# Expert rows in tiles of 128 + 96, the 96 as 32-column matmuls four side by side, and h's bound from sums that the relu accumulates

## The chip, the cores and the metric
The kernel runs on one core of one Trainium2 chip. Its time is the device time of an execution in microseconds (us). Engines are named as the profile names them: PE (TensorE), ACT (ScalarE), DVE (VectorE), POOL (GpSimd), SP (SyncE). They run side by side and wait for each other by semaphores only.

## The reference
Attention over 4 x 12 heads of 448 tokens gives x with 1792 rows of 768. A feed-forward layer (2048 wide, squared relu) gives y. A gate assigns each of the 1792 tokens to one of 8 experts, in order of falling logits, each expert taking exactly 224 rows. The part that changes is the last one:

```
for e in range(E):                      # E = 8
    mask = assigned == e                # 224 rows
    h = np.maximum(x[mask] @ w1[e], 0.0)    # 224 x 768 by 768 x 1024
    out[mask] = h @ w2[e]                   # 224 x 1024 by 1024 x 768
```

## The kernel before
Every float32 product is made of three float16 ones: an operand is scaled by a power of two, rounded (its hi part, on ACT) and the rest kept (its lo part, on DVE), and hi*hi + hi*lo + lo*hi is summed in PSUM. A scale needs a bound of the operand over all partitions, which POOL forms by a reduction over partitions (L656 to L667).

The expert stage is a loop that every engine writes out by itself: `step(e)` for e = -2, -1 and 0, a hardware loop for 1 to 5, then 6 and 7. Each engine's queue is in order. A turn overlaps three experts:
- PE (`step` at the end): `expert_up(e+1)`, L1742, 4 groups of 36 matmuls of 224 columns, each group followed by a relu; `expert_down(e, 0)` and `(e, 1)`; `turn_rows(e+2)`, 12 transposes; `expert_down(e, 2)` and `(e, 3)`. A down job, L1756, is 24 matmuls of 384 columns. The 224 rows are two tiles of 112, so job j is row tile j // 2 and column half j % 2. From its third group on, up waits for the relu two groups back, since it has two banks. A down needs all lo parts of h and of w2.
- ACT: `eh_hi(e)` (L850, after expert e-1's downs), `w2_hi(e)` (L859) with the relus of expert e+1 (L891) between, `w2_abs(e+1)` (L884, sums of w2's absolute values), `rows_out(0)` (L908, PSUM to the output tile), `w1_hi(e+2)` 0 and 1 (L866), `rows_out(1)`, `w1_hi` 2, `rows_hi(e+2)` (L871), `w1_hi` 3, `rows_out` 2 and 3.
- DVE: the lo parts `eh_lo(e)` (L1405) and `w2_lo(e)` (L1359); the absolute maximum of w1 of expert e+2 (L1354) and its scale (L343 to L355); the maximum of all of h of expert e+1 (L1436), which is read once POOL has reduced it, and its scale; `w1_lo(e+2)` 0 to 2 (L1364), `rows_lo(e+2)` (L1369), `w1_lo` 3; w2's scale (L1374 and three more); the output's scale o_inv (L1399). For expert 0 the maximum of h is taken in four parts (L1420), one per relu.
- POOL: the gather of expert e+2's rows (L650), the reductions for w1, w2 and h (L658, L661, L667), and two scatters of 112 output rows each (L674), one per row tile. SP loads w1 and w2, 3 MB each, two turns ahead.

The last expert's h and w2 parts lie where w1's were, so `eh_hi(7)` and `w2_hi(7)` don't wait for expert 6's downs: ACT does `rows_out(0)`, `eh_hi(7)`, `w2_hi(7)` 0 and 1, `rows_out(1)`, `w2_hi(7)` 2 and 3:

```
rows_out(0)
if is_last(e + 1):
    eh_hi(e + 1)
    w2_hi(e + 1, 0, 1)
...
rows_out(1)
if is_last(e + 1):
    w2_hi(e + 1, 2, 3)
```

Two earlier places matter for the prediction: the gate's matmuls (L1577) have 32 columns of weights and write four quarters of the partitions in turn, and one kind of tile in the layer before (L1651) has pairs of 64 columns.

Of the kernel before, what the change touches and what calls it, by code (L numbers as in the profile page):

```python
# [53 lines left out]
QK_ROWS = (TP, 128)  # L54
BEHIND = 2
# [11 lines left out]
def build(nc, q_d, k_d, v_d, cap_d, win_d, wout_d, wgate_d, w1_d, w2_d, out_d, y_d):  # L67
    with ExitStack() as ctx:
# [70 lines left out]
        grid = lambda: take(CH * E).rearrange("p (c e) -> p c e", e=E)  # L139
        masked, best, pick, newly, place = grid(), grid(), grid(), grid(), grid()  # L140
# [13 lines left out]
        low_hot = take(CH * TP // 2, F16).rearrange("p (c q) -> p c q", c=CH)  # L154
        group_hot = take(CH * CH).rearrange("p (c g) -> p c g", c=CH)
# [17 lines left out]
        lows = take(TP)  # L173
        grid_i = take(TP, I32)
# [24 lines left out]
        w1_sums, w1_tops, w2_sums, w2_tops, eh_parts_max, eh_tops = (take(4) for _ in range(6))  # L199
# [46 lines left out]
        BANK_E1, BANK_E2, BANK_ET = 0, 2, 4  # L246
# [31 lines left out]
        s_E2, s_o, s_oi, s_idx, s_sct, s_free = sem("expert_down"), sem("out_rows"), sem("out_inv"), sem("out_index"), sem("out_written"), sem("out_rows_free")  # L278
# [291 lines left out]
        def _(pool):  # L570
# [32 lines left out]
            pool.iota(grid_i, [[1, TP]], base=0, channel_multiplier=0).then_inc(s_rt, 1)  # L603
# [38 lines left out]
            def gather_rows(e):  # L642
                hold(s_tT, 3 * e)
                pool.tensor_copy(row_idx[0:TP], ids[0:TP, bass.ds(2 * e, 2)]).then_inc(s_gidx, 1)
                hold(s_gidx, e + 1)
                if first(e):
                    for t in range(NTILE - 4, NTILE):
                        hold(s_yw[t % 4], y_written(t))
                for c in range(2):
                    pool.indirect_dma_start(out=yg[0:TP, c, :], out_offset=None, in_=y_d[:, :],  # L650
                                            in_offset=bass.IndirectOffsetOnAxis(ap=row_idx[0:TP, c:c + 1], axis=0)).then_inc(s_ygl[c], 16)

            def step(e):
# [8 lines left out]
                if expert_live(e + 1):  # L662
                    hold(s_em, 1 if first(e + 1) else e + 3)
                    if first(e + 1):
                        pool.partition_all_reduce(eh_tops, eh_parts_max, 128, RMAX).then_inc(s_ea, 1)
                    else:
                        pool.partition_all_reduce(eh_amax, eh_max, 128, RMAX).then_inc(s_ea, 1)  # L667
                if expert_live(e):
                    pool.tensor_copy(idx[0:TP], ids[0:TP, bass.ds(2 * e, 2)]).then_inc(s_idx, 1)
# [12 lines left out]
        def _(act):  # L682
# [155 lines left out]
            def step(e):  # L838
# [64 lines left out]
                def rows_out(j):  # L903
                    if expert_live(e):
# [3 lines left out]
                        act.activation(e_out[0:TP, j // 2, (j % 2) * (DM // 2):(j % 2 + 1) * (DM // 2)],  # L908
                                       psum[0:TP, BANK_E2 + j % 2, 0:DM // 2], ACT.Copy, scale=o_inv[0:TP]).then_inc(s_o, 1)
# [30 lines left out]
        def _(dve):  # L940
# [255 lines left out]

            total = [0]
# [147 lines left out]
            dve.tensor_copy(ids[0:TP], psum[0:TP, BANK_IDS, 0:CH]).then_inc(s_ids, 1)  # L1345
# [5 lines left out]
            def step(e):  # L1351
# [66 lines left out]
                def part_max(j):  # L1418
                    dve.wait_ge(s_ER, 2 + j + 1)
                    return dve.tensor_reduce(eh_parts_max[:, j:j + 1], eh[:, j * 2 * CAP:(j + 1) * 2 * CAP], AX.X, ALU.max)  # L1420

                if first(e + 1):
                    part_max(0)
                    w1_lo(e + 2, 0)
                    part_max(1)
                    rows_lo(e + 2)
                    w1_lo(e + 2, 1)
                    part_max(2)
                    w2_lo(e + 1, 0)
                    part_max(3).then_inc(s_em, 1)  # L1430
                    dve.wait_ge(s_ea, 1)
# [356 lines left out]
```

## Time and profile before

| | us |
|---|---|
| median of 3 runs (lowest, highest) | 1068.84 (1066.81, 1070.94) |
| the profiled execution | 1069.31 |
| its span | 1067.6 |
| attention, feed-forward and routing, up to about | 798 |
| from the first gather to up(0) | 801 to 810.7 |
| expert loop, turns 1 to 5, each | 30.6 |
| last down, start to end | 1043.87 to 1059.66 |

A row of a timeline is start, duration, engine, line and operation, what it writes and reads, how many instructions are merged, and in brackets the idle time in front of it and what ended it. Durations of single matmuls include the fill of the array; what a matmul costs in a stream is read from the starts.

### The profile page before, as it was taken

The numbers are of one execution on the slowest core, as the hardware profiler recorded it, in microseconds if no ns is written. First come the engines' busy times: TensorE is split into PE (matmuls) and PEld (weight loads), VectorE is DVE, ScalarE is ACT, GpSimd is POOL, SyncE is SP. The second block draws the span as 40 slices with busy tenths as digits, with TensorE's granted clock in tenths as the row PEclk, the third lists the DMA queues.
The fourth block names the chain that finished last, engine by engine and source line by source line (L and its number), as shares of the span: only waits on it lengthen the run. The fifth ranks groups of instructions, "written<-read, shape, count | busy, mean of one in ns | idle before, by whom it ended". The sixth has DMA issues, their size and how long they took to land.

```text
span 1067.6 us, 23565 instructions
## 1 busy us (share of the span) xinstructions
PE 1029.5 (96%) x8700; PEld 748.3 (70%) x8700; DVE 819.5 (77%) x1699; ACT 588.9 (55%) x942; POOL 197.2 (18%) x319
## 2 busy tenths in 40 slices
PE   6999999999999999999999999999987999999996
PEld 3444444444469999999976666666656889888895
DVE  5899998999967656665686667666678899999971
ACT  5888887898846233333461111313215688877791
POOL 3444443444320000000000000000001132212211
PEclk9999999999999999999999999999997999999999
DMA  3752211121034000000241040401048566677401
GB/s 93 206 148 54 66 54 52 53 60 53 18 110 137 2 1 2 2 1 2 90 150 31 16 149 16 149 16 31 16 148 278 179 234 231 249 270 286 158 14 52
DMA packets 66782, 103.44 MB, mean 97 GB/s; under 512 B 14480, under 2 KB 44432, under 8 KB 66704
## 3 DMA queue, kind: packets, MB, share of 16 engines
q1 hardware_dynamic: 64144, 91.34, 26.0%
q0 software_dynamic: 2560, 11.01, 3.4%
q8 instruction: 54, 0.88, 0.4%
q14 instruction: 24, 0.20, 0.1%
HBM read 91.32 MB, written 11.01 MB: 96 GB/s over the span
## 4 chain that ended last, share of the span: by engine, by line
PE 79%; DVE 11%; issue 5%; DMA 2%; ACT 1%; POOL 1%; DVEq 0%; SPq 0%; POOLq 0%; ACTq 0%
PE psum L1465 21%; PE psum L1648 17%; PE psum L1756 10%; PE psum L1742 8%; PE psum L1510 5%; PE psum L1495 4%; PE psum L1519 4%; DVE arena L1030 3%; PE psum L1651 3%; PE psum L1681 2%; DMA arena<-y_rows,arena 1%; PE psum L1539 1%; DVE arena L1022 1%; PE psum L1724 1%; PE psum L1577 1%
## 5 line engine op out<-in xcount | busy, mean ns | idle before, releaser
L1465 PE MATMUL psum<-arena 128*128 128x224 f16 x2304 | 224.2, 259 | 1.0 <-DVE arena L1002 1.0
L1465 PEld LDWEIGHTS psum<-arena 128*128 128x128 f16 x2304 | 219.8, 98 | 5.3 <-issue 2.4
L1648 PE MATMUL psum<-arena 128*128 128x384 f16 x1152 | 195.9, 326 | 0.0
L1648 PEld LDWEIGHTS psum<-arena 128*128 128x128 f16 x1152 | 107.7, 98 | 66.9 <-issue 0.8
L590 POOL TENSOR_SCALAR arena<-arena 128x448 f32<-128x448 f32 x168 | 105.4, 638 | 162.0 <-DVE arena L1012 161.9
L1756 PE MATMUL psum<-arena 128*112 128x384 f16 x768 | 127.1, 326 | 0.4 <-issue 0.4
L723 ACT ACTIVATE arena<-arena 128x448 f32<-128x448 f32 x168 | 125.6, 750 | 1.0 <-DVE arena L1032 1.0
L805 ACT ACTIVATE arena<-psum,arena 128x384 f32<-128x384 f32 x28 | 16.2, 580 | 186.5 <-PE psum L1648 144.4
L1742 PE MATMUL psum<-arena 128*128 128x224 f16 x1152 | 114.0, 262 | 3.8 <-DVE arena L1390 2.0
L1756 PEld LDWEIGHTS psum<-arena 128*112 128x112 f16 x768 | 99.3, 130 | 24.8 <-issue 0.7
L1742 PEld LDWEIGHTS psum<-arena 128*128 128x128 f16 x1152 | 111.5, 99 | 6.0 <-DVE arena L1390 2.4
L716 ACT ACTIVATE arena<-psum,arena 128x896 f32<-128x896 f32 x96 | 87.5, 912 | 45.8 <-PE psum L1495 27.9
L738 ACT ACTIVATE arena<-psum 128x448 f32<-128x448 f32 x64 | 34.7, 543 | 136.0 <-PE psum L1465 136.0
L1519 PEld LDWEIGHTS psum<-arena 128*128 128x128 f32 x576 | 61.9, 142 | 62.7 <-issue 37.5
L1495 PE MATMUL psum<-arena 64*128 64x448 f32 (+1 forms) x336 | 100.1, 603 | 4.9 <-ACT arena L716 2.2
L1030 DVE TENSOR_REDUCE arena<-arena 128x2 f32<-128x896 f32 x96 | 92.2, 961 | 9.9 <-ACT arena L716 9.8
L1510 PE MATMUL psum<-arena 128*64 128x448 f32 (+1 forms) x384 | 93.5, 568 | 0.0
L1051 DVE TENSOR_REDUCE arena<-arena 128x1 f32<-128x448 f32 x64 | 39.3, 615 | 61.2 <-ACT arena L738 61.1
L1519 PE MATMUL psum<-arena 128*128 128x128 f32 x576 | 84.5, 283 | 1.4 <-POOL arena L590 1.3
L1022 DVE COPY arena<-psum 128x896 f32<-128x896 f32 x72 | 78.2, 1087 | 0.7 <-PE psum L1519 0.4
L1495 PEld LDWEIGHTS psum<-arena 64*128 64x128 f32 (+1 forms) x336 | 27.2, 183 | 69.7 <-issue 58.3
L1364 DVE SCALAR_TENSOR_TENSOR arena<-arena 128x1536 f16<-128x1536 f16 (+1 forms) x32 | 56.8, 1812 | 1.3 <-ACT arena L866 1.0
(236 smaller groups left out, 1379.0 us busy)
## 6 DMA issues: line engine op xcount, KB each, us to landing
arena<-moe_w SPq DMA_DIRECT2D x16, 3072.0 KB, 12.4
arena<-moe_w_out SPq DMA_DIRECT2D x32, 384.0 KB, 3.8
arena<-moe_w_in SPq DMA_DIRECT2D x16, 384.0 KB, 4.6
arena<-q SPq DMA_DIRECT2D x24, 224.0 KB, 2.7
arena<-v SPq DMA_DIRECT2D x24, 192.0 KB, 2.4
arena<-k SPq DMA_DIRECT2D x24, 96.0 KB, 2.6
arena<-k SPq DMA_DIRECT2D x48, 48.0 KB, 2.4
y_rows<-arena SPq DMA_DIRECT2D x4, 336.0 KB, 2.4
```

Of the source, the lines that this page charges most:

```text
L590: pool.tensor_scalar(prob[slot][:, h], prob[slot][:, h], p_rs[slot][:, h:h + 1], 1.0, ALU.mult, ALU.mult).then_inc(s_Pn, 2 // n)
L716: act.activation(prob[slot][:, 0:n], psum[:, BANK_S:BANK_S + n, 0:S], ACT.Tanh, scale=rcap_t).then_inc(s_T, 1)
L723: act.activation(prob[slot][:, h], prob[slot][:, h], ACT.Exp, bias=p_nb[slot][:, h:h + 1], scale=cap_t, accum_out=p_sum[slot][:, h:h + 1]) ...
L1022: dve.tensor_copy(pT[slot].rearrange("p h k q -> p (h k) q")[:, 0:NC + NKEY, cc * WIDE:(cc + 1) * WIDE], prob_T_of(bank).rearrange("p (j q ...
L1030: dve.tensor_reduce(p_max[slot][:, 0:n], prob[slot][:, 0:n], AX.X, ALU.max).then_inc(s_mx, 1)
L1465: last = pe.matmul(out, w_split[:, f, z, k * 128:(k + 1) * 128], x[u % 2][:, k, :], start=(k == 0 and m == 0), stop=(k == KD - 1 and m == 2))
L1495: last = pe.matmul(out, qT[slot][rows, columns], kT[slot][rows], start=True, stop=True)
L1510: last = pe.matmul(psum[D * h:D * h + D, BANK_X, 0:S], v_rows[slot][rows, column:column + D], keys_T, start=(kc == 0), stop=(kc == NKEY))
L1519: last = pe.transpose(out[:, j * WIDE:(j + 1) * WIDE], P_of[:, j * WIDE:(j + 1) * WIDE], ident)
L1648: last = pe.matmul(psum[:, BANK_Y + q % 4, 0:HALF], g_pair(p)[:, x, k, i * 128:(i + 1) * 128], w_split[:, k, z, columns], **flags)
L1742: last = pe.matmul(out, w[:, k, f * 128:(f + 1) * 128], x[:, k, :], start=(k == 0 and m == 0), stop=(k == KD - 1 and m == 2))
L1756: last = pe.matmul(psum[0:TP, BANK_E2 + j % 2, 0:DM // 2], h[:, k, c * TP:(c + 1) * TP], w[:, k, cols], start=(k == 0 and m == 0), stop=(k ...
```

## The change
- An expert's 224 rows become tiles of 128 and 96 rows. Jobs 2 and 3 are the column halves of the 128 rows. Job 0 is 64 of the 96 rows, both halves: two groups of 32 rows by two halves, four matmuls of 32 columns of weights that write four quarters of the partitions. Job 1 is the last 32 rows: the four quarters are two halves of the columns by two halves of the sum over k. Job 1 has bank 7 for itself.
- The two half sums of job 1 meet in a new function on DVE, `rows_sum`. ACT's `rows_out` 0 and 1 are now two instructions each.
- The relu also gives sums over its columns; their maximum over partitions takes the place of the maximum of h, for all experts.
- `rows_lo` on DVE and `rows_hi` on ACT move ahead of the third part of w1. The scatter of the 96 rows goes first.
- Tables of the routing that held 112 positions hold 128.

```diff
 QK_ROWS = (TP, 128)
+FULL = 128
+SLOTS = (FULL, CAP - FULL)
...
-        BANK_E1, BANK_E2, BANK_ET = 0, 2, 4
+        BANK_E1, BANK_ET = 0, 4
+        BANK_E2 = (2, 7, 3, 2)
...
-                    pool.indirect_dma_start(out=yg[0:TP, c, :], out_offset=None, in_=y_d[:, :],
-                                            in_offset=bass.IndirectOffsetOnAxis(ap=row_idx[0:TP, c:c + 1], axis=0)).then_inc(s_ygl[c], 16)
+                    pool.indirect_dma_start(out=yg[0:SLOTS[c], c, :], out_offset=None, in_=y_d[:, :],
+                                            in_offset=bass.IndirectOffsetOnAxis(ap=row_idx[0:SLOTS[c], c:c + 1], axis=0)).then_inc(s_ygl[c], 16)
...
                 if expert_live(e + 1):
-                    hold(s_em, 1 if first(e + 1) else e + 3)
-                    if first(e + 1):
-                        pool.partition_all_reduce(eh_tops, eh_parts_max, 128, RMAX).then_inc(s_ea, 1)
-                    else:
-                        pool.partition_all_reduce(eh_amax, eh_max, 128, RMAX).then_inc(s_ea, 1)
+                    hold(s_ER, 4 * (e + 2) + 2)
+                    pool.partition_all_reduce(eh_tops, eh_sums, 128, RMAX).then_inc(s_ea, 1)
...
-                for c in range(2):
+                for done, c in ((1, 1), (3, 0)):
                     if expert_live(e):
-                        hold(s_o, 4 * e + 2 * c + 4)
-                        pool.indirect_dma_start(out=out_d, out_offset=bass.IndirectOffsetOnAxis(ap=idx[0:TP, c:c + 1], axis=0),
-                                                in_=e_out[0:TP, c, :], in_offset=None).then_inc(s_sct, 16)
+                        hold(s_o, 3 * e + done + 2)
+                        if c == 1:
+                            hold(s_os, e + 2)
+                        pool.indirect_dma_start(out=out_d, out_offset=bass.IndirectOffsetOnAxis(ap=idx[0:SLOTS[c], c:c + 1], axis=0),
+                                                in_=e_out[0:SLOTS[c], c, :], in_offset=None).then_inc(s_sct, 16)
...
                     if expert_live(e + 1):
                         wait(act, s_E1, 4 * (e + 1) + j + 1)
                         wait(act, s_eL, 2 * (e + 1))
-                        act.activation(eh[:, j * 2 * CAP:(j + 1) * 2 * CAP], psum[:, BANK_E1 + j % 2, 0:2 * CAP], ACT.Relu).then_inc(s_ER, 1)
+                        act.activation(eh[:, j * 2 * CAP:(j + 1) * 2 * CAP], psum[:, BANK_E1 + j % 2, 0:2 * CAP], ACT.Relu,
+                                       accum_out=eh_sums[:, j:j + 1]).then_inc(s_ER, 1)
...
                         wait(act, s_E2, 4 * e + j + 2)
                         wait(act, s_oi, e + 1)
                         wait(act, s_free, e + 1)
-                        act.activation(e_out[0:TP, j // 2, (j % 2) * (DM // 2):(j % 2 + 1) * (DM // 2)],
-                                       psum[0:TP, BANK_E2 + j % 2, 0:DM // 2], ACT.Copy, scale=o_inv[0:TP]).then_inc(s_o, 1)
+                        source = psum[:, BANK_E2[j], 0:HALF]
+                        if j >= 2:
+                            act.activation(e_out[:, 0, (j % 2) * HALF:(j % 2 + 1) * HALF], source, ACT.Copy, scale=o_inv).then_inc(s_o, 1)
+                            return
+                        rows = slice(0, 64) if j == 0 else slice(64, 96)
+                        for n in range(2):
+                            part = slice(64 * n, 64 * n + 64 - 32 * j)
+                            last = act.activation(e_out[rows, 1, n * HALF:(n + 1) * HALF], source[part], ACT.Copy, scale=o_inv[part])
+                        last.then_inc(s_o if j == 0 else s_op, 1)
...
                 if steady:
+                    rows_hi(e + 2)
                     w1_hi(e + 2, 2)
-                    rows_hi(e + 2)
                     w1_hi(e + 2, 3)
                 rows_out(2)
                 rows_out(3)
...
             for h in range(2):
                 half = slice(h * CH // 2, (h + 1) * CH // 2)
-                dve.tensor_tensor(low_hot[0:TP, half], low_of[0:TP, half].unsqueeze(2).broadcast_to([TP, CH // 2, TP]),
-                                  lows[0:TP].unsqueeze(1).broadcast_to([TP, CH // 2, TP]), ALU.is_equal).then_inc(s_hot, 1)
+                dve.tensor_tensor(low_hot[0:TP, half], low_of[0:TP, half].unsqueeze(2).broadcast_to([TP, CH // 2, FULL]),
+                                  lows[0:TP].unsqueeze(1).broadcast_to([TP, CH // 2, FULL]), ALU.is_equal).then_inc(s_hot, 1)
...
+                def rows_sum(e):
+                    wait(dve, s_op, e + 1)
+                    for n in range(2):
+                        part, rows = slice(64 * n + 32, 64 * n + 64), e_out[64:96, 1, n * HALF:(n + 1) * HALF]
+                        last = dve.scalar_tensor_tensor(rows, psum[part, BANK_E2[1], 0:HALF], o_inv[part], rows, ALU.mult, ALU.add)
+                    last.then_inc(s_os, 1)
+
                 def up_lo(e):
                     for j in range(3):
+                        if j == 2 and not first(e):
+                            rows_lo(e)
+                            if expert_live(e - 2):
+                                rows_sum(e - 2)
                         w1_lo(e, j)
                     if first(e):
                         w1_lo(e, 3)
@@ -1391,11 +1414,11 @@
                                                             ALU.mult, ALU.subtract)
                         last.then_inc(s_ygL, 1)
                         return
-                    rows_lo(e)
                     w1_lo(e, 3)
...
                 def rows_scale(e):
-                    wait(dve, s_o, 4 * e + 2)
+                    wait(dve, s_o, 3 * e + 2)
+                    wait(dve, s_os, e + 1)
                     dve.tensor_tensor(o_inv, o_part, w2_inv, ALU.mult).then_inc(s_oi, 1)
...
                 if is_last(e):
                     rows_scale(e)
+                    rows_sum(e)
...
-                def part_max(j):
-                    dve.wait_ge(s_ER, 2 + j + 1)
-                    return dve.tensor_reduce(eh_parts_max[:, j:j + 1], eh[:, j * 2 * CAP:(j + 1) * 2 * CAP], AX.X, ALU.max)
-
                 if first(e + 1):
-                    part_max(0)
                     w1_lo(e + 2, 0)
-                    part_max(1)
                     rows_lo(e + 2)
                     w1_lo(e + 2, 1)
-                    part_max(2)
                     w2_lo(e + 1, 0)
-                    part_max(3).then_inc(s_em, 1)
-                    dve.wait_ge(s_ea, 1)
-                    dve.tensor_reduce(eh_amax, eh_tops, AX.X, ALU.max).then_inc(s_em, 1)
-                    dve.wait_ge(s_em, 2)
-                elif expert_live(e + 1):
-                    wait(dve, s_ER, 4 * (e + 2) + 2)
-                    dve.tensor_reduce(eh_max, eh, AX.X, ALU.max).then_inc(s_em, 1)
                 if expert_live(e + 1):
                     wait(dve, s_ea, e + 2)
+                    dve.tensor_reduce(eh_amax, eh_tops, AX.X, ALU.max).then_inc(s_em, 1)
+                    wait(dve, s_em, e + 2)
                     pow2_scale(dve, eh_amax, eh_inv, eh_scl, s_ee, 4 * (e + 1))
                     dve.tensor_tensor(o_part, eh_inv, w1_y, ALU.mult).then_inc(s_ee, 1)
                     wait(dve, s_ee, 4 * (e + 2))
@@ -1449,6 +1461,8 @@
                 if expert_live(e + 1):
                     if not first(e + 1):
                         w2_scale(e + 1)
+                    if is_last(e + 1):
+                        rows_sum(e)
                     if not is_last(e + 1):
                         rows_scale(e + 1)
...
             def expert_down(e, j):
-                c, half = j // 2, j % 2
                 wait(pe, s_eL, 2 * (e + 1))
                 wait(pe, s_w2L, 4 * (e + 1))
-                wait(pe, s_o, 4 * e + j + 1)
+                if j == 1:
+                    wait(pe, s_os, e + 1)
+                else:
+                    wait(pe, s_o, 3 * e + (2, 2, 2, 3)[j])
+                pe.sem_inc(s_pe, 1)
                 hh, hl = (x.rearrange("p (k t) -> p k t", k=KE) for x in eh_parts(e))
                 wH, wL = (w.rearrange("p (k n) -> p k n", k=KE) for w in w2_parts(e))
-                for k in range(KE):
-                    cols = slice(half * (DM // 2), (half + 1) * (DM // 2))
-                    for m, (h, w) in enumerate(((hh, wH), (hh, wL), (hl, wH))):
-                        last = pe.matmul(psum[0:TP, BANK_E2 + j % 2, 0:DM // 2], h[:, k, c * TP:(c + 1) * TP], w[:, k, cols],
-                                         start=(k == 0 and m == 0), stop=(k == KE - 1 and m == 2))
+                terms = [(k, h, w) for k in range(KE) for h, w in ((hh, wH), (hh, wL), (hl, wH))]
+                half = len(terms) // 2
+                out = psum[:, BANK_E2[j], 0:HALF]
+                if j >= 2:
+                    for t, (k, h, w) in enumerate(terms):
+                        last = pe.matmul(out, h[:, k, 0:FULL], w[:, k, (j % 2) * HALF:(j % 2 + 1) * HALF],
+                                         start=(t == 0), stop=(t == 2 * half - 1))
+                for t in range((2 * half, half)[j] if j < 2 else 0):
+                    for group in range(4):
+                        n, r = group // 2, group % 2
+                        k, h, w = terms[t + half * r * j]
+                        first_slot = FULL + 32 * (2 if j else r)
+                        last = pe.matmul(out[32 * group:32 * group + 32], h[:, k, first_slot:first_slot + 32], w[:, k, n * HALF:(n + 1) * HALF],
+                                         start=(t == 0), stop=(t == (2 * half, half)[j] - 1))
                 last.then_inc(s_E2, 1)
```

## Rows read from the trace of the kernel before

**Rows 1.** The page, part 1: busy time, share of span, instructions, by engine.

```profile
PE 1029.5 (96%) x8700; PEld 748.3 (70%) x8700; DVE 819.5 (77%) x1699; ACT 588.9 (55%) x942; POOL 197.2 (18%) x319
```

**Rows 2.** Windows, one turn: length, busy time by engine, granted clock, DMA share, GB/s.

```profile
922.40:953.00 30.60, 30.60 (x255) 27.46 (x254) 28.20 (x27) 25.02 (x28) 7.33 (x9) 1.00 0.68 250
```

**Rows 3.** Chain of waits in order of time (start, us, what): a turn, the last down.

```profile
891.83 13.80 PE psum L1742 x144
905.63 7.80 PE psum L1756 x48
913.43 1.15 PE psum L1724 x12
...
1043.87 15.79 PE psum L1756 x96
```

**Rows 4.** Timeline of PE: the gate's rounds of four, and pairs of 64 columns.

```profile
383.75 0.96 PE L1577 MATMUL psum<-arena 128*32 128x224 f16 x32
384.64 0.56 PE L1465 MATMUL psum<-arena 128*128 128x224 f16 x4
...
600.38 7.99 PE L1651 MATMUL psum<-arena 128*64 128x384 f16 x96
608.21 0.46 PE L1681 MATMUL psum<-arena 112*64 112x8 bf16 x10
```

**Rows 5.** Timeline of DVE, then of ACT, in one turn of the loop.

```profile
922.70 0.15 DVE L1374 TENSOR_REDUCE arena<-arena 128x1 f32<-128x4 f32 x1
...
924.01 2.21 DVE L1405 SCALAR_TENSOR_TENSOR arena<-arena 128x896 f16<-128x896 f32 x2 [0.41 <-ACT arena L850]
926.59 7.00 DVE L1359 SCALAR_TENSOR_TENSOR arena<-arena 128x1536 f16<-128x1536 f16 x4 [0.38 <-ACT arena L859]
933.52 6.54 DVE L1354 TENSOR_REDUCE arena<-arena 128x1 f32 x1
...
941.24 2.02 DVE L1436 TENSOR_REDUCE arena<-arena 128x1 f32<-128x1792 f32 x1
...
944.80 5.28 DVE L1364 SCALAR_TENSOR_TENSOR arena<-arena 128x1536 f16<-128x1536 f16 x3
949.99 1.61 DVE L1369 SCALAR_TENSOR_TENSOR arena<-psum,arena 128x1344 f16<-128x1344 f32 x1
...
924.82 3.02 ACT L859 ACTIVATE arena<-arena 128x1536 f16 x2
927.75 0.52 ACT L891 ACTIVATE arena<-psum 128x448 f32<-128x448 f32 x1
...
941.38 3.04 ACT L866 ACTIVATE arena<-arena 128x1536 f16 x2 [0.68 <-DVE arena L355]
944.34 0.56 ACT L908 ACTIVATE arena<-psum,arena 112x384 f32<-112x384 f32 x1
...
946.26 1.36 ACT L871 ACTIVATE arena<-psum,arena 128x1344 f16<-128x1344 f32 x1
```

**Rows 6.** Timeline of DVE in the first steps of the expert stage.

```profile
829.23 0.62 DVE L1420 TENSOR_REDUCE arena<-arena 128x1 f32<-128x448 f32 x1 [0.46 <-ACT arena L891]
...
842.45 6.54 DVE L1354 TENSOR_REDUCE arena<-arena 128x1 f32<-128x6144 f32 x1
```

**Rows 7.** Timeline of ACT in step 6, from the last relu on.

```profile
1027.88 0.54 ACT L891 ACTIVATE arena<-psum 128x448 f32<-128x448 f32 x1 [1.28 <-PE psum L1742]
...
1033.29 1.98 ACT L850 ACTIVATE arena<-arena 128x896 f16<-128x896 f32 x2 [0.93 <-DVE arena L1440]
...
1038.10 0.56 ACT L908 ACTIVATE arena<-psum,arena 112x384 f32<-112x384 f32 x1
```

**Rows 8.** Windows around PE's idle time before the experts; the clock stands third from the end.

```profile
801.00:805.00 4.00, 0.00 (x0) 0.00 (x0) 4.00 (x4) 0.00 (x0) 2.74 (x2) 0.55 0.38 97
...
810.70:812.00 1.30, 1.30 (x8) 1.05 (x9) 1.30 (x1) 1.30 (x2) 0.99 (x2) 0.50 1.04 421
...
815.00:816.00 1.00, 1.00 (x12) 0.99 (x11) 1.00 (x1) 0.56 (x1) 0.00 (x0) 0.96 0.95 277
```

More of the change, by code:

```diff
@@ L139, in build @@
         grid = lambda: take(CH * E).rearrange("p (c e) -> p c e", e=E)
+        group_hot = view(at[0], CH * CH).rearrange("p (c g) -> p c g", c=CH)
+        assert CH * CH <= 2 * CH * E
         masked, best, pick, newly, place = grid(), grid(), grid(), grid(), grid()
@@ L153, in build @@
         at[0] = X_ODD
-        low_hot = take(CH * TP // 2, F16).rearrange("p (c q) -> p c q", c=CH)
-        group_hot = take(CH * CH).rearrange("p (c g) -> p c g", c=CH)
+        low_hot = take(CH * FULL // 2, F16).rearrange("p (c q) -> p c q", c=CH)
         group_tok = take(CH * CH // 2, F16).rearrange("p (c g) -> p c g", c=CH)
@@ L172, in build @@
         groups, tok = take(CH), take(CH)
-        lows = take(TP)
-        grid_i = take(TP, I32)
+        lows = take(FULL)
+        grid_i = take(FULL, I32)
         tok_i = take(CH, I32)
@@ L198, in build @@
         ym, y2_inv, y2_scl = take(1), take(1), take(1)
-        w1_sums, w1_tops, w2_sums, w2_tops, eh_parts_max, eh_tops = (take(4) for _ in range(6))
+        w1_sums, w1_tops, w2_sums, w2_tops, eh_sums, eh_tops = (take(4) for _ in range(6))
         sel_blocks = take(BLK)
@@ L277, in build @@
         s_E1, s_ER, s_em, s_ea, s_ee, s_eH, s_eL = sem("expert_up"), sem("expert_relu"), sem("eh_max"), sem("eh_amax"), sem("eh_scale"), sem("eh_hi"), sem("eh_lo")
-        s_E2, s_o, s_oi, s_idx, s_sct, s_free = sem("expert_down"), sem("out_rows"), sem("out_inv"), sem("out_index"), sem("out_written"), sem("out_rows_free")
+        s_op, s_os = sem("out_rows_part"), sem("out_rows_sum"); s_E2, s_o, s_oi, s_idx, s_sct, s_free = sem("expert_down"), sem("out_rows"), sem("out_inv"), sem("out_index"), sem("out_written"), sem("out_rows_free")
         s_wgl = sem("gate_loaded")
@@ L602, in _ @@
             pool.iota(w8_i.bitcast(I32), [[-1, E]], base=E, channel_multiplier=0).then_inc(s_rt, 1)
-            pool.iota(grid_i, [[1, TP]], base=0, channel_multiplier=0).then_inc(s_rt, 1)
+            pool.iota(grid_i, [[1, FULL]], base=0, channel_multiplier=0).then_inc(s_rt, 1)
             pool.iota(tok_i.rearrange("p (b c) -> p b c", b=B)[0:TP], [[S, B], [1, NC]], base=0, channel_multiplier=NC).then_inc(s_rt, 1)
@@ L643, in gather_rows @@
                 hold(s_tT, 3 * e)
-                pool.tensor_copy(row_idx[0:TP], ids[0:TP, bass.ds(2 * e, 2)]).then_inc(s_gidx, 1)
+                pool.tensor_copy(row_idx, ids[:, bass.ds(2 * e, 2)]).then_inc(s_gidx, 1)
                 hold(s_gidx, e + 1)
@@ L1195, in _ @@
             row_scales()
+            dve.sem_inc(s_os, 1)
             total = [0]
@@ L1333, in _ @@
             emit(dve.tensor_reduce(pair_of[0:TP], newly[0:TP], AX.X, ALU.add))
-            link(dve.tensor_scalar(half_of[0:TP], rank[0:TP], float(TP), None, ALU.is_ge))
+            link(dve.tensor_scalar(half_of[0:TP], rank[0:TP], float(FULL), None, ALU.is_ge))
             emit(dve.tensor_tensor(group_of[0:TP], pair_of[0:TP], half_of[0:TP], ALU.add))
-            link(dve.scalar_tensor_tensor(low_of[0:TP], half_of[0:TP], -float(TP), rank[0:TP], ALU.mult, ALU.add))
+            link(dve.scalar_tensor_tensor(low_of[0:TP], half_of[0:TP], -float(FULL), rank[0:TP], ALU.mult, ALU.add))
             link(dve.tensor_tensor(group_hot[0:TP], group_of[0:TP].unsqueeze(2).broadcast_to([TP, CH, CH]),
@@ L1712, in _ @@
                     pe.wait_ge(s_hot, 2 + c // (CH // 2))
-                last = pe.matmul(psum[0:TP, BANK_IDS, 0:CH], low_hot[0:TP, c, :], group_tok[0:TP, c, :], start=(c == 0), stop=(c == CH - 1))
+                last = pe.matmul(psum[:, BANK_IDS, 0:CH], low_hot[0:TP, c, :], group_tok[0:TP, c, :], start=(c == 0), stop=(c == CH - 1))
             last.then_inc(s_idm, 1)
@@ L1723, in turn_rows @@
                     for k in range(KD):
-                        last = pe.transpose(psum[:, BANK_ET + k // 2, (k % 2) * CAP + c * TP:(k % 2) * CAP + (c + 1) * TP],
-                                            yg[0:TP, c, k * 128:(k + 1) * 128], ident[0:TP, 0:TP])
+                        n, base = SLOTS[c], (k % 2) * CAP + c * FULL
+                        last = pe.transpose(psum[:, BANK_ET + k // 2, base:base + n], yg[0:n, c, k * 128:(k + 1) * 128], ident[0:n, 0:n])
                         if c == 1 and k % 2 == 1:
```

4 lines of the change are left out of this document (2 added, 2 removed).

## Prediction

> **What bounds the kernel now.** The page comes first: PE is busy 96% of the span, DVE 77%, ACT 55% [rows 1]. Those shares mix stages, and the change touches only the experts, so the windows are read next: in one turn of the expert loop (30.6 us) PE has no idle time at all, but DVE is busy 28.2 and ACT 25.0 [rows 2]. The chain of waits then gives the turn's terms: up 13.80, two down jobs 7.80, turned rows 1.15, two more down jobs 7.80, together 30.55 [rows 3]. So PE is the bound, with DVE 2.4 us behind, and most of those 2.4 us are round trips between engines, not slack. A cut on PE is worth what it takes off only until DVE's loop closes; hence the timeline of DVE and ACT inside a turn [rows 5], and those of the ends [rows 6, 7], where nothing hides anything.
>
> **PE, what goes.** Before, four jobs of 24 matmuls of 384 columns: 7.80 / 48 = 0.1625 us each, 15.6 in all. After, jobs 2 and 3 keep 24 each (128 rows cost what 112 do, since the 384 columns stream), 7.80. Jobs 0 and 1 are 24 and 12 rounds of four 32-column matmuls. What is a round worth? Pairs of 64-column matmuls of the same 384 columns ran at (608.21 - 600.38) / 48 = 0.163 us a pair: side by side is free. The gate has true rounds of four, with 224 columns: 0.89 us for 8 rounds [rows 4], against 8 x 13.80 / 144 = 0.77 for full ones, 0.12 over. As one cost per burst this is 0.12 per expert, as a surcharge per round 15 ns, 0.55 per expert. I take the first, since pairs show none per round: 36 x 0.1625 + 0.13 = 5.98 in place of 7.8, 1.8 us less per expert. PE's turn becomes 28.73. The two new waits in front of a job, and its sem_inc, wait for things done long before, and are costed at nothing.
>
> The Trainium skill has a rule that speaks against this: "TensorE: Matmul & The Clock Gate", section "Measured speedup vs the span model", gives three column tiles side by side a speedup of 2.38, so a round costs 1.26 single matmuls (an estimate from that page: 205 ns). The gate's row, 111 ns against 96, shows 1.16 at most, with the burst's ends in it. "TensorEngine Tiling (Array Packing)", section "Key Properties", says that changing the mode drains the engine; the 0.12 us per burst fits that.
>
> **DVE's loop, the new bound.** I walk from T, the start of what follows w1's scale (941.24 before) [rows 5]. Going out: the 2.02 us maximum of eh and the 0.59 us trip to POOL behind it (POOL now reduces the relu's sums, ready about 4 us earlier). Coming in: a 0.19 us maximum of four numbers, and rows_sum, two instructions of 384 columns from PSUM, 0.54 each by rows_lo's rate (1.61 us for 1344, plus start; bounds 0.4 and 0.7). New order:
> - ACT starts w1_hi at T+0.14, two of them 2.96; rows_out(1) is now two instructions at 0.46 spacing (944.34 to 944.80), 0.92; rows_hi 1.36: done T+5.4.
> - DVE: six small ones (scale of eh), then w1_lo(0) waits for w1_hi(0), T+1.74; two w1_lo 3.46 (5.19 for three): T+5.2; rows_lo waits for rows_hi, T+5.4 to 6.95; rows_sum to 8.0; two w1_lo to 11.5; w2's scale, four small ones at 0.19: W = T+12.2; o_inv to 12.4; eh_lo 2.2 to 14.6; four w2_lo 6.93 (926.59 to 933.52) to 21.55; the reduce of w1 and its scale 7.72 (933.52 to 941.24): T+29.3.
> So DVE's turn is 29.3 us (between 28.9 and 29.8 by the bounds above), over PE's 28.73. DVE doesn't stall PE by rows_lo (ready 1.4 us early), but by ACT: relu(0) stands behind two w2_hi, which wait for W. PE's third group of up goes on at W + 0.05 + 2.93 (924.82 to 927.75) + 0.62 (relu 0.52, accumulator about 0.1) + 0.15 = W+3.75, and up ends E = W+3.75+6.9 = W+10.65. ACT's additions (two rows_out 0.92, four accumulator reads 0.4) fit its 5.6 us of idle time per turn, except the 0.92 ahead of rows_hi, counted. The extra PE cost, if rounds were 15 ns dearer, hides in the 0.57 us by which DVE is late.
>
> **The start.** Part maxima leave: POOL's reduce comes after relu(3) and not after the maximum, 0.62 us earlier [rows 6] (bounds 0.4 to 0.8). The first reduce of line 1354 then starts at 841.83, T = 849.55, W(1) = 861.8. W(6) = 861.8 + 5 x 29.3 = 1008.2, E of the last up = 1018.9, where it was 1027.7: 8.8 us gained by then. Routing's one-hot table grows from 112 to 128 columns, 0.3 us; the gather behind it waits for the y rows anyway; nothing.
>
> POOL's scatters swap: the 96 rows go first and wait for rows_sum (T+8), the 128 rows wait for rows_out(3), as the last scatter did before. Behind them in POOL's queue stand the next gather and w1's reduce; the gather is wanted by PE some 20 us later, the reduce waits for DVE anyway: nothing. Moving rows_hi ahead of w1_hi(2) is in the walk.
>
> **The end, where it is given back.** DVE's rows_sum(6) stands before eh_lo(7) and waits for rows_out(1) of expert 6. ACT issues that one only after eh_hi(7) and two w2_hi(7) (1038.10) [rows 7]; before, DVE could start eh_lo(7) on the first half of eh_hi. After: relu(3) at E+0.2; eh_hi 5.41 later (1027.88 to 1033.29), plus 0.1 and 0.19 for accumulator and reduce: E+5.9; eh_hi and w2_hi 4.81 (1033.29 to 1038.10), E+10.7; rows_out(1) twice 1.04, rows_sum 1.1: E+12.9; eh_lo 2.2, w2_lo 7.0, w2L ready: E+22.3. Without that wait E+16.5; before about E+16.2. PE ends expert 6 at E+13.8 and idles 8.5 us. An idle of this length has a price: where PE stood idle for the first gather, the granted clock was down to 0.55, and when dense matmuls began at 810.7 it was still 0.50 (1.2 GHz), up to 0.96 at 815 [rows 8]: 4.3 us at half speed, 2.15 lost (bounds 0, and 5 if the turn to full speed comes as late as after the sparse transposes of 805 to 815).
>
> The last down starts at 1018.9 + 22.3 = 1041.2 (before 1043.87), takes 13.78 + 2.15, ends 1057.1. From there to the span's end 7.94 stays (1067.6 less 1043.87 + 15.79), with the 128-row scatter last: the span is 1065.0, 2.6 less. The profiled execution took 1069.31 (span 1067.6 and 1.7 around it), so 1066.7; that execution is 0.5 over the median of 1068.84. I say 1066.6.
>
> **Rivals.**
> 1. The wait for rows_sum(6) doesn't show (rows_out(1) comes earlier than I read). Then E+16.5, PE idles 2.7 us, too short I think for the clock to fall: 5.8 + 2.15 less, 1058.7, faster. For it: only that such waits are sometimes hidden; against: the order on ACT in rows 7, unchanged by the diff.
> 2. DVE's loop is shorter than PE's (relu sums so early that the trips vanish): turn 28.73, 5 x 0.55 = 2.8 less, 1063.9. For it: DVE's busy time falls to about 27.2 in a turn; against: w1's scale, w1_hi(0), w1_lo(0) is a pure chain.
> 3. Slower: rounds of four are dear, since four short weight loads and four different streams share what one had. Place: jobs 0 and 1 of every expert. PE's turn is 22.9 + 36r; from r = 178 ns it passes DVE's, at 188 ns all the gain is gone, from 209 the kernel is over 0.5% slower. With the four loads beside and not under the stream (0.7 us for 32 loads, 88 ns a round, r = 250): five turns of 2.6, 2.0 at the start, 3.2 in the last down, 18.2 in all, 1084.9. Against: the gate's 111 ns holds stream and loads.
> By the 205 ns of the Trainium skill ("TensorE: Matmul & The Clock Gate"), PE's turn would be 30.3 and the time 1073.7, 0.4% slower.
> 4. The tiles don't run together at all: 144 matmuls in a row, 17.5 us per expert more, over 1190. Only the gate's row speaks on it, against.
>
> **How the numbers follow.** Forecast 0.58, rival 1 0.12, rival 2 0.13, rival 3 0.12, rival 4 0.01, others 0.04. Of rival 3's chance 0.05 lies at the price of the Trainium skill's clock-gate page, 205 ns. About 0.5% (5.3 us) is what can be told from no change. The forecast's own range: DVE's turn +-0.4 times five, clock price 0 to 4, rounds +0.5: 1062 to 1071. With rival 1 outside below, and the part of rival 3 over 200 ns a round outside above: 1060 to 1072. Faster (below 1063.5): rival 1, a third of rival 2, the low tail of the forecast: 0.28. Slower (over 1074.2): half of rival 3, rival 4, some mishap: 0.10. Within: 0.62.
>
> **What would show it.** Down's first two jobs together 6.0 us in the chain; turns of 29.3 with a PE stall near 0.6 us, released by line 891's relu; up(7) over near 1019; a gap of about 8.5 us before the last down, ended by DVE's w2_lo, with a half-speed clock after. Wrong if the first jobs take over 6.4 us, if turns are 28.7 or over 29.8, or if that gap is under 5 us.

## The result and the profile after

The changed kernel takes 1070.95 us (median of 20 executions, 1069.42 to 1072.23) against 1068.69 for the kernel before: ratio 1.0022, interval 1.0015 to 1.0028. It is slower by 0.2%. That is less than the half per cent that the chances set as "no change", but it is clear of the noise, and on the other side of the forecast, which was 2 us less. The profiled execution took 1071.67 us with a span of 1070.0, where 1065.0 was forecast.

The page and the windows first. The page's line answers to [rows 1], the window to [rows 2]:

```profile
PE 1017.6 (95%) x9468; PEld 715.6 (67%) x9468; DVE 815.2 (76%) x1711; ACT 602.3 (56%) x990; POOL 204.8 (19%) x319
```
```profile
921.00:951.40 30.40, 28.99 (x350) 23.21 (x348) 27.60 (x29) 26.61 (x33) 9.13 (x9) 1.00 0.69 252
```

In a window the numbers are its length, then busy time and count of PE, PE's weight loads, DVE, ACT and POOL, then PE's granted clock. PE has lost 12 us of work, yet the turn of the loop is nearly as long as before, 30.4 us against 30.55: PE now idles 1.4 us in it. The timeline of PE says where, and what a round of four costs:

```profile
926.20 7.07 PE L1756 MATMUL psum<-arena 128*128 128x224 f16 x72 [1.41 <-ACT arena L894]
933.20 6.04 PE L1782 MATMUL psum<-arena 128*32 128x384 f16 x144
939.16 1.37 PE L1739 MATMUL psum<-arena 128*128 128x128 f32 x12
940.37 7.96 PE L1775 MATMUL psum<-arena 128*128 128x384 f16 x48
```

The 36 rounds take 939.16 - 933.20 = 5.96 us (5.98 forecast). Their starts lie 162 to 163 ns apart, and 0.1 us is left per burst. The rounds are as good as hoped; the third group of up waits for a relu. That relu stands behind DVE's chain, as the same turn's rows of DVE and then ACT show; they answer to [rows 5]:

```profile
922.52 0.16 DVE L1422 TENSOR_TENSOR arena<-arena 128x1 f32<-128x1 f32 x1 [0.21 <-DVE arena L359]
923.03 2.22 DVE L1428 SCALAR_TENSOR_TENSOR arena<-arena 128x896 f16<-128x896 f32 x2 [0.35 <-issue]
925.16 7.00 DVE L1371 SCALAR_TENSOR_TENSOR arena<-arena 128x1536 f16<-128x1536 f16 x4
932.08 6.55 DVE L1366 TENSOR_REDUCE arena<-arena 128x1 f32 x1
...
941.64 3.55 DVE L1376 SCALAR_TENSOR_TENSOR arena<-arena 128x1536 f16<-128x1536 f16 x2 [0.52 <-ACT arena L869]
945.63 1.62 DVE L1381 SCALAR_TENSOR_TENSOR arena<-psum,arena 128x1344 f16<-128x1344 f32 x1 [0.44 <-ACT arena L874]
947.28 1.25 DVE L1394 SCALAR_TENSOR_TENSOR arena<-psum,arena 32x384 f32<-32x384 f32 x2
948.57 3.55 DVE L1376 SCALAR_TENSOR_TENSOR arena<-arena 128x1536 f16<-128x1536 f16 x2
952.03 0.15 DVE L1386 TENSOR_REDUCE arena<-arena 128x1 f32<-128x4 f32 x1
...
922.49 3.04 ACT L862 ACTIVATE arena<-arena 128x1536 f16 x2 [1.59 <-DVE arena L359]
925.44 0.52 ACT L894 ACTIVATE arena<-psum 128x448 f32<-128x448 f32 x1
...
943.04 1.16 ACT L919 ACTIVATE arena<-psum,arena 32x384 f32<-32x384 f32 x2
944.22 1.38 ACT L874 ACTIVATE arena<-psum,arena 128x1344 f16<-128x1344 f32 x1
```

ACT waits 1.59 us for w2's scale (L359), DVE for nothing longer than 0.63 in the whole turn: DVE sets it. And the end, ACT, DVE and PE from the last up on, which answers to [rows 7]:

```profile
1024.32 6.03 PE L1782 MATMUL psum<-arena 128*32 128x384 f16 x144
1030.13 1.98 ACT L853 ACTIVATE arena<-arena 128x896 f16<-128x896 f32 x2 [0.51 <-DVE arena L1452]
1032.01 3.03 ACT L862 ACTIVATE arena<-arena 128x1536 f16<-128x1536 f32 x2
1035.07 1.15 ACT L919 ACTIVATE arena<-psum,arena 32x384 f32<-32x384 f32 x2
1036.32 1.25 DVE L1394 SCALAR_TENSOR_TENSOR arena<-psum,arena 32x384 f32<-32x384 f32 x2 [5.47 <-ACT arena L919]
1037.60 2.22 DVE L1428 SCALAR_TENSOR_TENSOR arena<-arena 128x896 f16<-128x896 f32 x2
1039.73 7.00 DVE L1371 SCALAR_TENSOR_TENSOR arena<-arena 128x1536 f16<-128x1536 f32 x4
1046.84 7.60 PE L1782 MATMUL psum<-arena 128*32 128x384 f16 x144 [8.58 <-DVE arena L1371]
```

DVE stands idle for 5.47 us in front of rows_sum(6), released by rows_out(1), and PE for 8.58 in front of the last down, whose first two jobs take 7.60 us, where the same jobs of expert 6 took 6.03. The windows show the granted clock at 0.50 for the first 3 us, and `warm` below tests whether that is the reason. They answer to [rows 8]:

```profile
1046.80:1047.80 1.00, 0.96 (x16) 0.58 (x20) 0.01 (x1) 0.00 (x0) 0.00 (x0) 0.50 0.00 0
...
1050.80:1051.80 1.00, 1.00 (x32) 0.70 (x24) 0.00 (x0) 0.00 (x0) 0.00 (x0) 1.00 0.06 16
```

### The profile page after: what moved, and what is told of

Read it like the earlier page. It is cut to its first block, busy times and chain, and to the rows that moved or that the text cites. A ratio compares the mean times of both kernels' runs of the same rounds, so it can differ in the third digit from the quotient of the medians.

```text
span 1070.0 us, 25202 instructions
## 1 busy us (share of the span) xinstructions
PE 1017.6 (95%) x9468; PEld 715.6 (67%) x9468; DVE 815.2 (76%) x1711; ACT 602.3 (56%) x990; POOL 204.8 (19%) x319
## 4 chain that ended last, share of the span: by engine, by line
PE 66%; DVE 17%; issue 9%; ACT 5%; DMA 2%; POOL 1%; DVEq 0%; ACTq 0%; SPq 0%; POOLq 0%
PE psum L1479 21%; PE psum L1662 17%; PE psum L1524 6%; PE psum L1509 5%; PE psum L1533 5%; DVE arena L1366 4%; PE psum L1665 3%; DVE arena L1371 3%; ACT arena L869 3%; DVE arena L1041 3%; DVE arena L1376 2%; PE psum L1695 2%; PE psum L1553 2%; DMA arena<-y_rows,arena 1%; PE psum L1756 1%
## 5 line engine op out<-in xcount | busy, mean ns | idle before, releaser
L1662 PE MATMUL psum<-arena 128*128 128x384 f16 x1152 | 195.9, 326 | 0.0
L1756 PE MATMUL psum<-arena 128*128 128x224 f16 x1152 | 114.7, 261 | 10.2 <-ACT arena L894 8.1
L1775 PE MATMUL psum<-arena 128*128 128x384 f16 x384 | 63.7, 326 | 0.0
L1782 PE MATMUL psum<-arena 128*32 128x384 f16 x1152 | 49.8, 333 | 8.6 <-DVE arena L1371 8.6
```

Of the source, the lines that this page charges most:

```text
L1662: last = pe.matmul(psum[:, BANK_Y + q % 4, 0:HALF], g_pair(p)[:, x, k, i * 128:(i + 1) * 128], w_split[:, k, z, columns], **flags)
L1756: last = pe.matmul(out, w[:, k, f * 128:(f + 1) * 128], x[:, k, :], start=(k == 0 and m == 0), stop=(k == KD - 1 and m == 2))
```

## The experiments

**One half of the change alone.** `sums_only` is the kernel before with the new bound; `tiles_only` is the changed kernel with the old bound, the maxima on DVE:

```diff
 # sums_only, against the kernel before
-psum[:, BANK_E1 + j % 2, 0:2 * CAP], ACT.Relu)
+psum[:, BANK_E1 + j % 2, 0:2 * CAP], ACT.Relu, accum_out=eh_sums[:, j:j + 1])
...
-    dve.tensor_reduce(eh_max, eh, AX.X, ALU.max)
...
 # tiles_only, against the changed kernel: the same lines the other way
```

> The kernel before with only the bound changed: the relu accumulates sums, the maxima of h leave DVE, the tiles stay 112 + 112. Theory (corrected walk): PE stays the bound with turns of 30.55 us and no idle time in them, DVE gets about 2.3 us of slack per turn; only the start moves, up(2) begins about 1.7 us earlier (0.6 from the first reduce, and the 0.9 us stall goes), and the end gives back 0.3: 1.4 us less than before, 1067.3. Rival (the accumulator reads on ACT delay the relus that PE waits for): turns over 30.7, slower than before by 1 us or more.

> The changed kernel with the old bound: tiles of 128 + 96, rounds of four and rows_sum, but DVE takes the maxima of h again. Theory (DVE and ACT close the turn): each turn grows by about 1.3 us over the changed kernel's 30.4, to 31.7 (2.6 us for maximum and trip come in, of which the waits for w1_hi and rows_hi, 1 us, and the small maximum hide some), 1.3 and 0.6 at the start: about 8 us over the changed kernel, 1079. Rival (PE or its tiles set the turn of 30.4): no more than 1 us over the changed kernel.

Measured: `sums_only` 1066.64 us, ratio to before 0.9981 (0.9973 to 0.9990); `tiles_only` 1080.71, 1.0105 (1.0091 to 1.0120). `sums_only` was expected at 1067.3; in it the chain is PE's without a stall, 30.55 a turn:

```profile
981.37 13.80 PE psum L1728 x144
995.17 7.80 PE psum L1742 x48
1002.97 1.15 PE psum L1710 x12
1004.12 7.80 PE psum L1742 x48
1011.92 13.80 PE psum L1728 x144
```

In `tiles_only` two o_inv lie 31.78 us apart on DVE (31.7 expected):

```profile
928.80 0.16 DVE L1424 TENSOR_TENSOR arena<-arena 128x1 f32<-128x1 f32 x1 [0.21 <-DVE arena L359]
...
960.58 0.16 DVE L1424 TENSOR_TENSOR arena<-arena 128x1 f32<-128x1 f32 x1 [0.21 <-DVE arena L359]
```

The turns are as the theory had them, but the kernel lost 9.8 us against the changed one, not 8. The theory left out the clock: twice in the loop, at 870 and at 965.5, it stood at 0.50 for 3.4 us in this profile, and one second half of up took 8.72 us in place of 7.06; around the last down it was 10.2 us.

So the sums alone gain 2 us, at the start, and the tiles alone lose 11: taking 1.7 us of a turn from PE and putting 1.3 on DVE makes the kernel slower as soon as DVE is over PE. Only with the sums does the change come within 0.2% of the kernel before.

**The end.** `late_sum` moves one call:

```diff
-if is_last(e + 1): rows_sum(e)      # before eh_lo(7)
...
 if is_last(e):
+    rows_sum(e - 1)                 # after w2_lo(7)
     rows_scale(e)
```

> The changed kernel, with rows_sum of expert 6 moved on DVE from before eh_lo(7) to after w2_lo(7). Theory (the wait for rows_out(1) behind eh_hi(7) and w2_hi(7) on ACT makes the gap at the end): the last down starts 16.6 us after up(7) ends in place of 22.5, PE's gap falls from 8.6 to about 2.8 us, its clock holds and the last down loses none of its 1.65 us: 7.4 us less than the changed kernel, 1063.5, below the kernel before. Rival (the gap is w2_lo(7)'s own chain): under 1.5 us less.

Measured 1064.34 us, ratio to before 0.9959 (0.9947 to 0.9971), 6.6 less than the changed kernel. The rows of DVE and PE:

```profile
1031.14 2.21 DVE L1428 SCALAR_TENSOR_TENSOR arena<-arena 128x896 f16<-128x896 f32 x2 [0.42 <-ACT arena L853]
...
1041.31 1.25 DVE L1394 SCALAR_TENSOR_TENSOR arena<-psum,arena 32x384 f32<-32x384 f32 x2
1041.38 4.63 PE L1781 MATMUL psum<-arena 128*32 128x384 f16 x103 [3.25 <-DVE arena L1371]
1046.26 1.96 PE L1781 MATMUL psum<-arena 128*32 128x384 f16 x41 [0.26 <-issue]
```

The last down starts 17.2 us after up ends (1024.18), where it was 22.6 and 16.6 was expected: one call placed before a wait cost more than the 3.4 us that the change had gained by the end of up(7). The expectation was 7.4 us less. The 0.8 that is missing shows in the second row of PE. The clock stayed at 1.00, yet the first two jobs took 6.77 us (next start at 1048.15) and not 5.96, because PE paused for about 0.7 us two rounds into job 1. No semaphore is waited for at that place, and the profile names no cause. The scatter of the 96 rows was moving data then (DMA share 0.62); whether it had to do with the pause, no run tests.

`warm` fills the wait in the changed kernel instead, with 48 matmuls whose result nobody reads:

```diff
+if is_last(e + 1):                  # behind the downs of expert 6
+    for k in range(48):
+        pe.matmul(psum[:, BANK_ET, 0:HALF], w2H[:, 0:128], w2L[:, 0:HALF], start=True, stop=True)
```

> The changed kernel with 48 matmuls of 384 columns, whose result nobody reads, behind the downs of expert 6, so that PE works through 7.8 of its 8.6 us of waiting. Theory (the 1.6 us that the first two jobs of the last down take over 5.98 are the clock's): these two jobs take 6.0 us, the granted clock stays 1.0 through the last down, 1.6 us less than the changed kernel, 1069.3, and its two groups of times, 1069.5 and 1071.7, become one. Rival (PE pays for its instruction stream or the tile mode there): they still take over 7 us.

Measured 1069.56 us, ratio 1.0006 (0.9997 to 1.0014) where the changed kernel had 1.0022. In the profile the first two jobs fell to 6.0 us:

```profile
1049.04 6.03 PE L1782 MATMUL psum<-arena 128*32 128x384 f16 x144 [0.78 <-issue]
```

So the 1.6 us were the clock's. The second half of the expectation failed: the times did not draw together (1068.33 to 1072.34). The mean granted clock of each execution is known too. In the changed kernel it was 0.989 in the ten under 1070.7 us and 0.986 to 0.988 in the ten over 1071.2, so the two groups differ in time at half clock. One place of that kind lies far ahead of the experts, in attention, which the change leaves alone. The clock stood at 0.50 from 162.6 to 166.0 us in the changed kernel's profile, from 161.7 to 168.5 in that of `warm`, and not at all there in those of `best2`, `best4` and `no_sum`. Each 3.4 us of it moved everything behind it by 1.1 to 1.6 us, whatever the edit. Which place makes the changed kernel's two groups stays open, since only one of its executions was profiled.

**The turn.** `hi_first` puts rows_hi ahead of rows_out(1) on ACT; `no_sum` leaves out the second half sum's addition for expert rows 192 to 223; `dve_unrolled` writes DVE's steps 1 to 5 out.

```diff
 # hi_first
+if steady: rows_hi(e + 2)
 rows_out(1)
...
 # no_sum, in rows_sum
-for n in range(2): ... dve.scalar_tensor_tensor(rows, psum[part, ...], o_inv[part], rows, ...)
+dve.sem_inc(s_os, 1)
 # dve_unrolled
-expert_steps(dve, step)
+for e in range(-2, E): step(e)
```

> The changed kernel, with ACT's rows_hi moved ahead of rows_out(1), so that the now two instructions of rows_out(1) no longer stand before it. Theory (one chain on DVE from w1's scale on): DVE's wait of 0.43 us for rows_hi goes in every turn, six times, 2.5 us less than the changed kernel, 1068.4, turns of 30.0. Rival (the turn is closed by the relu behind w2_hi on ACT, whatever DVE does): turns stay 30.4.

> The changed kernel with the two instructions of rows_sum left out (the second half sum of expert rows 192 to 223 is not added); the wait for rows_out(1) in front of them stays. Theory (everything on DVE's chain counts in full while it is over PE's 28.8): the turn falls by the 1.29 us that rows_sum takes on it, 30.4 to 29.1, PE's stall in the turns to about 0.3 us each, and the last down starts 1.3 us sooner after up(7): 9 us less than the changed kernel, 1062. Rival (the turn is closed elsewhere, at ACT or at the relus): under 3 us less.

> The changed kernel with the steps 1 to 5 written out on DVE only, the other engines keep their loop. Theory (the 0.35 us in front of eh_lo that is put down to issue is DVE's own loop end, now on the chain): turns of 30.07 in place of 30.42, five times, 1.7 us less than the changed kernel, 1069.2. Rival (the 0.35 us is the wait for eh_hi's semaphore): no difference.

Measured: `hi_first` 1068.90 us, ratio 1.0004 (0.9995 to 1.0013); `no_sum` 1062.12, 0.9942 (0.9923 to 0.9960); `dve_unrolled` 1068.05, 0.9996 (0.9985 to 1.0006). Against the changed kernel these are 2.1, 8.8 and 2.9 us less, where 2.5, 9 and 1.7 were expected. Each edit shortens the turn of 30.43 by what it takes off DVE's chain. In `hi_first` rows_lo follows w1_lo without a wait, and the turn, eh_lo to eh_lo (921.55 to 951.57), is 30.02:

```profile
940.16 3.55 DVE L1377 SCALAR_TENSOR_TENSOR arena<-arena 128x1536 f16<-128x1536 f16 x2 [0.52 <-ACT arena L869]
943.74 1.62 DVE L1382 SCALAR_TENSOR_TENSOR arena<-psum,arena 128x1344 f16<-128x1344 f32 x1
```

In `no_sum` rows_lo comes every 940.09 - 911.03 = 29.06 us. In `dve_unrolled` not only the 0.35 us in front of eh_lo went but also the 0.21 in front of o_inv, 29.81 a turn:

```profile
921.79 0.16 DVE L1422 TENSOR_TENSOR arena<-arena 128x1 f32<-128x1 f32 x1
921.86 2.21 DVE L1428 SCALAR_TENSOR_TENSOR arena<-arena 128x896 f16<-128x896 f32 x2
```

Both gaps need the loop, but they are not one thing. In the kernel before, o_inv stood in the same loop with one wait in front of it, and it followed w2's scale (923.25) without a gap:

```profile
923.44 0.16 DVE L1399 TENSOR_TENSOR arena<-arena 128x1 f32<-128x1 f32 x1
```

The change put a second wait there, for rows_sum, and in the loop the 0.21 us came with it. No run takes this wait out alone.

**A version better than both.** `best2` joins `late_sum`, `hi_first` and `dve_unrolled` with one more edit:

```diff
+if expert_live(e + 1) and not first(e + 1):
+    w2_scale(e + 1)                 # behind w1's scale
 if expert_live(e + 1):
     wait(dve, s_ea, e + 2)          # then h's scale
...
-if not first(e + 1): w2_scale(e + 1)   # behind the last w1_lo
```

> The changed kernel with four edits: rows_sum(6) behind w2_lo(7), rows_hi ahead of rows_out(1), DVE's steps written out, and w2's scale on DVE right behind w1's scale, where DVE waits for POOL and for w1_hi (0.75 us of small instructions move into 0.75 us of idle time). Theory: turns of 30.4 less 0.43, 0.35 and about 0.55, so 29.1, still 0.3 over PE's; 7 us in the turns and 6.6 at the end less than the changed kernel: 1057.4, 1% under the kernel before. Rival (PE's instruction stream or ACT closes the turn next): turns stay over 29.7, 1061 or more.

Measured 1057.12 us, ratio to before 0.9886 (0.9869 to 0.9902): 1.1% faster than before (1057.4 was expected, with turns of 29.1). The chain is PE's again, 28.87 a turn, with nothing between the rows:

```profile
914.07 13.80 PE psum L1756 x144
927.87 5.96 PE psum L1782 x144
933.84 1.30 PE psum L1739 x12
935.14 7.80 PE psum L1775 x48
942.94 13.80 PE psum L1756 x144
```

Its last down still began at a low clock in the profile, after a wait of 3.65 us. `best3` adds 20 idle-time matmuls there, as in `warm`; `best4` also puts some into the wait for the first gather:

```diff
 last.then_inc(s_idm, 1)
+for k in range(30):
+    pe.matmul(psum[:, BANK_POS, 0:128], ident, ident, start=True, stop=True)
```

> The kernel with four edits (1057.1), and 20 matmuls of 384 columns whose result nobody reads in the 3.6 us in which PE waits before the last down. Theory (in the profile of the four edits this wait took the clock to 0.50, and the last down's first two jobs took 8.76 us and not 5.98): these jobs take 6.0 us, 2.8 us less, 1054.4. Rival (the clock falls anyway, by how dense the stretch is, or the wait was short in most executions): under 1 us less.

> As best3, and 30 float32 matmuls of 128 columns (about 6.4 us) in the 8.0 us in which PE waits for the first gather. Theory: the clock stays at 1.0 where it was 0.50 from 801 to 815, the first six transposes behind the second gather take 0.7 us and not 1.4 and the first half of up(0) 6.9 us and not 9; the part behind them is held by DVE's maximum of w1 and the second gather, so no more than 0.7 to 2 us of it arrive at the end: 1053.0. Rival (DVE and the gathers set all of that stretch): the same as best3 within 0.3 us.

Measured: `best3` 1056.61 us, 0.9887 (0.9872 to 0.9902), no different from `best2`; `best4` 1059.07, 0.9916 (0.9902 to 0.9929), worse. Both expectations of a gain failed (1054.4 and 1053.0). First the last down of `best2`, then that of `best3`:

```profile
1031.99 8.76 PE L1782 MATMUL psum<-arena 128*32 128x384 f16 x144 [3.65 <-DVE arena L1372]
```
```profile
1032.57 4.54 PE L1782 MATMUL psum<-arena 128*32 128x384 f16 x103 [0.40 <-issue]
1037.35 1.95 PE L1782 MATMUL psum<-arena 128*32 128x384 f16 x41 [0.24 <-issue]
```

In these two executions the two jobs fell from 8.7 to 6.7 us and not to 6.0: at a clock of 1.00, `best3` has the same pause of 0.7 us two rounds into job 1 as `late_sum`. And `best2`'s profile is of its slowest execution (1057.97 of 1056.10 to 1057.97), with a mean granted clock of 0.988; its two fastest had 0.991. The 6.8 us at half clock before and in the last down are worth 0.003 of that mean, so the fast ones probably lost little or nothing there, and the filling had nothing to give back to them. No trace of one is there to show it.

In `best4` the clock held at 1.0 while the matmuls ran. It was back at 0.50 from 805.4 on, after a wait of PE of 2.95 us, and still there for up(0):

```profile
797.00:801.00 4.00, 4.00 (x39) 4.00 (x38) 3.70 (x7) 0.00 (x0) 0.23 (x2) 1.00 0.18 58
...
810.70:815.00 4.30, 4.12 (x23) 3.34 (x24) 4.30 (x2) 4.30 (x4) 1.14 (x2) 0.50 1.05 425
```

Why it is 2.5 us slower than `best3` shows on POOL, in the gather's wait for the rows of y to be written, first `best3`, then `best4`:

```profile
800.64 1.68 POOL L654 DMA_INDIRECT arena<-y_rows,arena  x1 [2.17 <-DMA y_rows<-arena]
```
```profile
801.23 1.58 POOL L654 DMA_INDIRECT arena<-y_rows,arena  x1 [4.00 <-DMA y_rows<-arena]
```

The last write of y took 4.33 us from issue to landing beside the filling matmuls, and 2.48 to 2.51 in the profiles of all other kernels, so the gather started 1.8 us later than it could. In the profiles alone `best4` is only 0.9 us longer than `best3`, since its own had kept the clock in attention, which put it 1.2 us ahead there. Why the write takes longer beside these matmuls, no run shows.

## Why the prediction was right and wrong

Right, with the measured number behind:
- The rounds of four: 5.98 forecast, 5.96 measured. The dear rounds of rival 3 did not come. The Trainium skill ("TensorE: Matmul & The Clock Gate", section "Measured speedup vs the span model") measured a speedup of 2.38 for three column tiles, by estimate 1.26 single matmuls a round. This stream does not bear it out: four tiles cost 1.00.
- The start: w2's scale of expert 1 was done at 861.9 (861.8 forecast).
- What closes the turn: DVE, by way of w2's scale, two w2_hi and the relu in front of PE's third group; up(7) ends 10.66 us after W (10.65 forecast).
- The end: last down 22.6 us after up(7) (22.3), PE's idle time 8.58 (8.5), the clock's price 1.6 (2.15), the tail 7.66 (7.94).

**The step that failed** is the sum "So DVE's turn is 29.3 us (between 28.9 and 29.8 by the bounds above)". It was 30.43, beyond the 29.8 that the prediction itself named as the sign of being wrong. The mechanism was right, DVE's chain closes the turn, and every large term in it; five small ones were short, all of them joins between instructions. `hi_first`, `no_sum` and `dve_unrolled` took three of them out one at a time, and the turn fell by 0.41, 1.37 and 0.62 us. From T = 939.82, and forecast against measured:
- w1_hi and then rows_out(1): 3.10 and 3.22, 0.1.
- rows_out(1), two instructions of 32 rows each: each taken at the 0.46 us spacing of one large instruction and its unlike successor, measured 1.18 for the pair (943.04 to 944.22) against 0.92, 0.26 more. It stands before rows_hi, so DVE waits for it; `hi_first` took this out.
- rows_lo, from its start to that of rows_sum: 1.55 and 1.65, 0.10. In `no_sum`, where a w1_lo follows it, the same instruction takes 1.57.
- rows_sum: 1.08 and 1.29, 0.21. The pair did not overlap either.
- o_inv and the loop's end: 0.19 and 0.72 (from w2's scale done, 922.31, to eh_lo, 923.03), 0.53. Before, the 0.41 us in which eh_lo waited for ACT [rows 5] covered the loop's end, and I read this wait as ACT's alone. The second wait in front of o_inv was in the diff and not in the sum. `dve_unrolled` shows both: 0.62 a turn.

Together 1.2 us, of which 0.1 came back, mostly in eh_lo, and this five times, the first turn being 0.5 shorter: W(6) came at 1013.6 and not at 1008.2, up(7) ended at 1024.2 and not at 1018.9. With 5.3 more there, 0.3 more to the last down, 0.4 less in it and 0.3 less behind it, 1065.0 becomes 1069.9; 1070.0 was measured. Two slips stand beside this and change nothing. PE's own turn was taken at 28.73 us with 1.15 for the turned rows, which in tiles of 128 and 96 take 1.30 (`best2`: 28.87). And a span of 1065.0 gives 1066.7 for the profiled execution and 1066.2 for the median, and the forecast says 1066.6.

The sign follows from that one term: the turn saved 0.13 us of 30.55 in place of 1.25, so that the start's gain and the turns' together (3.4 us at the end of up(7)) were less than what the end takes back: the last down starts 22.6 us after up(7) where it started 16.2 after it, and at its low clock it is hardly shorter (15.5 us, before 15.8). The bounds on the turn were too narrow because they were put on rows_sum and not on each join between two instructions. Rival 1 held 2.7 us of idle time too short for the clock to fall; `tiles_only` lost the clock after a wait of 1.98 us, so that argument was weak, though the case never arose.

## What to carry to other kernels

Where two engines are close to each other, here within 2.4 us in a turn of 30.6, taking work from the first is worth only the distance to the second, and the second's chain has to be walked with every join in it: spacing between instructions of the same kind, waits, and the end of a hardware loop, which was free as long as something else was waited for. Four edits that take time off the new bound or off the end (w2's scale and rows_hi moved into waits, the loop on DVE written out, rows_sum(6) moved back) made the changed kernel 1.1% faster than the kernel before, and about 0.9% faster than `sums_only`. No run has these edits without the tiles; but the turn of `sums_only` is PE's own work without a stall, 30.55 us, and of all the edits only the tiles take work from PE. And a helper that waits for another engine must not stand in front of the last chain of the kernel: one call cost 6.6 us.

## What the runs showed of the hardware

- Four matmuls of 32 weight columns over 384 columns each ran side by side at 162.5 ns a round, what one full matmul takes, with 0.1 us per burst of 144.
- Two ACT instructions of 384 columns and 32 or 64 rows, each reading PSUM, took 1.16 to 1.17 us as a pair, where one of 112 or 128 rows took 0.56 to 0.58: splitting by rows doubled the time. The pair of 128 rows in `rows_out(2)` and `(3)` overlapped by 0.1 us (1.04 for both); these pairs did not.
- The hardware loop cost DVE 0.6 us a turn where DVE is what the turn waits for (30.43 to 29.81): 0.35 between the last instruction of one turn and the first of the next, and 0.21 in front of an instruction with two waits.
- The length of one wait of PE does not tell whether the clock falls. It fell to 0.50 with waits of 3.65 us (`best2`), 2.95 (`best4`) and 1.98 (`tiles_only`, once in the loop), and held through one of 3.25 in `late_sum`. Filling the wait before the last down with matmuls kept it at 1.0 (`warm`, `best3`); filling the first 7 us of the wait for the gather did not help the dense work that came 8 us after the filling ended.
- In `late_sum` and `best3`, PE paused for 0.7 us in the middle of a burst of matmuls, with no wait on a semaphore and the clock at 1.00. The cause is open.
